# First batch of a fused attention, expert and mixing kernel: the gates of part 0 go through all their steps alone, parts 1 and 2 follow between the first masks, and a weight product moves behind the first increments

## The reference

```python
f = 1.0 / (1.0 + np.exp(-f_logit))                     # layer 1: gated linear attention
state = f[:, :, t, :, None] * state + einsum('bhd,bhe->bhde', k[:, :, t], v[:, :, t])
y[:, :, t] = einsum('bhd,bhde->bhe', q[:, :, t], state)
...
# layer 2: 4 experts of causal softmax attention (q, k, v of width 64), top 2 of 4 per token
# layer 3: theta = x @ w_theta; y = w_tok_r @ (x cos theta) + w_tok_i @ (x sin theta)
#          u = x + y; out = u + relu(u @ w_ch)
```

## Time and profile before

| | |
|---|---|
| median of 3 runs | 611.98 us (611.74 to 612.78) |
| profiled execution, its own time | 614.31 us |
| its span | 612.6 us, mean granted TensorE clock 0.989 |
| PE busy | 569.5 us, 93% of the span |
| DVE, ACT, POOL busy | 61%, 49%, 21% |
| chain that ended last | PE 77%, ACT 10%, DVE 8% |

### The profile page before, as it was taken

How to read it: one execution, slowest core, us unless ns; L and a number is a source line. 1 busy time by engine, 2 the same in 40 slices (tenths; PEclk the granted TensorE clock), 3 DMA queues, 4 the chain that set the end, 5 groups by cost and what they waited for, 6 DMA issues and landing times.

```text
span 612.6 us, 13201 instructions
## 1 busy us (share of the span) xinstructions
PE 569.5 (93%) x5532; PEld 526.5 (86%) x5532; DVE 376.0 (61%) x695; ACT 301.3 (49%) x623; POOL 127.5 (21%) x87
## 2 busy tenths in 40 slices
PE   0979899989899998999998989999999999999997
PEld 0779778889678987888996879999999999999997
DVE  2977868667776686766476757755344543455324
ACT  5658586645667366653357736523341233224211
POOL 1003440402340004400022314701320131012210
PEclk9999999999999998999998989999999999999999
DMA  8937020043110070000520000001000100010002
GB/s 284 308 114 285 26 53 27 2 137 150 53 53 2 7 281 0 2 1 4 217 95 1 2 1 1 1 2 69 10 1 1 51 27 1 1 52 27 0 1 78
DMA packets 17966, 37.19 MB, mean 61 GB/s; under 512 B 2160, under 2 KB 10608, under 8 KB 17392
## 3 DMA queue, kind: packets, MB, share of 16 engines
q1 hardware_dynamic: 17904, 36.32, 17.2%
HBM read 31.46 MB, written 4.72 MB: 59 GB/s over the span
## 4 chain that ended last, share of the span: by engine, by line
PE 77%; ACT 10%; DVE 8%; issue 2%; DMA 1%; SPq 0%; DVEq 0%; ACTq 0%
PE bank L1142 17%; PE bank L1143 17%; PE bank L1144 17%; PE bank L1341 5%; ACT prob L696 5%; PE bank L1368 4%; PE bank L1315 4%; PE bank L1160 3%; PE bank L1240 2%; DVE nmax L1043 2%; PE bank L1236 2%; PE bank L1207 1%; PE bank L1419 1%; PE bank L1221 1%; DMA gate<-fT 1%
## 5 line engine op out<-in xcount | busy, mean ns | idle before, releaser
L1142 PE MATMUL bank<-z_h,wt_h 128*128 128x384 f32 x288 | 98.1, 340 | 1.8 <-DVE z_l L871 1.8
L1143 PE MATMUL bank<-z_l,wt_h 128*128 128x384 f32 x288 | 97.8, 339 | 0.0
L1144 PE MATMUL bank<-z_h,wt_l 128*128 128x384 f32 x288 | 96.9, 337 | 0.0
L696 ACT ACTIVATE prob<-bank,nmax 128x384 f32<-128x384 f32 (+5 forms) x96 | 60.0, 631 | 28.4 <-DVE nmax L1043 28.3
L1043 DVE TENSOR_REDUCE nmax<-bank 128x1 f32<-128x384 f32 (+5 forms) x96 | 55.1, 619 | 27.1 <-PE bank L1321 19.6
L494 POOL TENSOR_TENSOR trig<-trig,x 128x768 f32<-128x768 f32 x18 | 33.5, 1862 | 152.1 <-ACT trig L588 92.7
L886 DVE TENSOR_SCALAR turns<-bank 128x384 int32<-128x384 f32 x22 | 12.2, 557 | 73.1 <-PE bank L1144 73.1
L1142 PEld LDWEIGHTS bank<-z_h,wt_h 128*128 128x128 f32 x288 | 54.1, 188 | 2.5 <-issue 2.2
L1143 PEld LDWEIGHTS bank<-z_l,wt_h 128*128 128x128 f32 x288 | 54.4, 189 | 0.0
L1144 PEld LDWEIGHTS bank<-z_h,wt_l 128*128 128x128 f32 x288 | 54.3, 189 | 0.0
L1341 PE MATMUL bank<-ident,prob 128*128 128x128 f32 x336 | 48.3, 290 | 4.5 <-ACT portion L711 3.9
(11 more groups left out here) (177 smaller groups left out, 1402.2 us busy)
## 6 DMA issues: line engine op xcount, KB each, us to landing
V<-v SPq DMA_DIRECT2D x4, 1152.0 KB, 10.1
gate<-fT SPq DMA_DIRECT2D x12, 384.0 KB, 3.2
q<-qT SPq DMA_DIRECT2D x12, 384.0 KB, 5.9
k<-kT SPq DMA_DIRECT2D x12, 384.0 KB, 6.4
wt_raw<-w_tok SPq DMA_DIRECT2D x6, 768.0 KB, 8.2
out<-x SPq DMA_DIRECT2D x24, 192.0 KB, 1.9
gate<-fT SPq DMA_DIRECT2D x3, 512.0 KB, 6.2
q<-qT SPq DMA_DIRECT2D x3, 512.0 KB, 9.6
```

What stands on the lines that cost most here:

```text
L696: nc.scalar.activation(prob[:, m % 2, r, at], bank[r][:, at], ACT.Exp, bias=nmax[:, m, k:k + 1], accum_out=den[:, m // 2, which, e:e + 1]) ...
L1142: nc.tensor.matmul(o, a_h, b_h, start=start, stop=False)
L1143: nc.tensor.matmul(o, a_h, b_l, start=False, stop=False)
L1144: return nc.tensor.matmul(o, a_l, b_h, start=False, stop=stop)
```

## The change

It reorders instructions on ACT, DVE and PE, and adds no arithmetic. ACT: part 0 goes through Exp and Ln alone; then Exp of part 1, Exp of minus the sum and Exp of the sum of part 0, Exp of part 2, Ln of parts 1 and 2; part 0's chunk decays come behind the first `kTs` copy, the rest of part 1 behind them. DVE: the scan of part 0 ahead of part 2's clamp; the scan of part 1 between the masks of chunks 0 and 1; q and k of part 1 and the scan of part 2 behind the first state; k of part 2 a chunk earlier. PE: `theta_weights` behind `turn_k(1)`, bank 5 first, bank 4 after ACT has copied the first outputs out of it. The second batch's clamps and Exps: two of four move from chunk 3 to chunk 4, the others behind the copies and splits of the transposed `xn`.

```diff
+            exp_first(0)
+            log_first(0)
+            exp_first(1)
             shrink_first(0)
             grow_first(0)
-            shrink_first(1)
-            act.wait_ge(wth_mm, 1)
-            nc.scalar.copy(staged(W_OTH, 768, 2), bank[2]...).then_inc(wth_copied, 1)
-            grow_first(1)
+            exp_first(2)
+            log_first(1)
+            log_first(2)
...
+                        if it < 1 and c == 0:      # ACT, behind the copy kTs of chunk c
+                            decay_chunks(chunks_of(0))
+                            shrink_first(1)
+                        if it < 1 and c == 2:
+                            shrink_first(2)
+                            grow_first(2)
...
                             if c == 1:             # ACT, behind the copy xn of chunk c - 1
-                                shrink_first(2)
-                                grow_first(2)
+                                grow_first(1)
+                                act.wait_ge(wth_mm, 1)
+                                nc.scalar.copy(staged(W_OTH, 768, 2), bank[2]...).then_inc(wth_copied, 1)
...
-                            elif c in (4, 5):
-                                exp_gates(it + 1, range(2 * c - 8, 2 * c - 6))
+                            elif c == NT - 1:
+                                exp_gates(1, (0, 1))
...
                         if it < 1:                 # ACT, behind the copies of the transposed xn
-                            log_gates(it + 1)
+                            exp_gates(1, (2, 3))
+                            log_gates(1)
...
+            clamp_first(0)                         # DVE
+            clamp_first(1)
             dve.wait_ge(consts, 13)
             scan_first(0)
-            scan_first(1)
+            clamp_first(2)
             scale_first_q(0)
             scale_first_k(0)
-            scale_first_q(1)
...
                 mask(0)
                 if it < 1:
-                    scale_first_k(1)
+                    scan_first(1)
...
                         if c == 0:                 # DVE, behind the state of chunk c
+                            scale_first_q(1)
+                            scale_first_k(1)
                             scan_first(2)
                         elif c == 1:
                             scale_first_q(2)
                             worst_sum(0)
-                        elif c == 2:
                             scale_first_k(2)
-                        elif c in (3, 4):
-                            clamp_gates(1, 2 * c - 6)
-                            clamp_gates(1, 2 * c - 5)
+                        elif c == NT - 2:
+                            clamp_gates(1, 0)
+                            clamp_gates(1, 1)
...
+                if it < 1:                         # DVE, behind the splits xT_l, ahead of the copies Vm
+                    clamp_gates(1, 2)
+                    clamp_gates(1, 3)
...
-            pe.wait_ge(w_in[3], 32)                # PE, ahead of scores(0, 0)
-            for a in range(2):
-                for c in range(NC):
-                    mm = theta_weights(a, c)
-            mm.then_inc(wth_mm, 1)
...
-                if it < 1:
-                    pe.wait_ge(wth_copied, 1)
                 outputs(0)
                 increments(0)
                 turn_k(1)
+                if it < 1:
+                    pe.wait_ge(w_in[3], 32)
+                    for a in (1, 0):
+                        if a == 0:
+                            pe.wait_ge(x_copied, 1)
+                        for c in range(NC):
+                            mm = theta_weights(a, c)
+                    mm.then_inc(wth_mm, 1)
```

More of the change, by code:

```diff
@@ L602, in grow_first, with exp_first, log_first @@
                 nc.scalar.activation(gate[:, :, part(n)], gate[:, :, part(n)], ACT.Exp).then_inc(grown, 1)
-                decay_chunks(chunks_of(n))
-            for n in range(PARTS):
+                if n >= 1:
+                    decay_chunks(chunks_of(n))
+            def exp_first(n):
                 act.wait_ge(clamped, n + 1)
                 nc.scalar.activation(gate[:, :, part(n)], gate[:, :, part(n)], ACT.Exp, scale=-1.0).then_inc(expf, 1)
-            for n in range(PARTS):
+            def log_first(n):
                 act.wait_ge(expf, n + 1)
                 nc.scalar.activation(gate[:, :, part(n)], gate[:, :, part(n)], ACT.Ln, bias=1.0).then_inc(logf, 1)
+            exp_first(0)
+            log_first(0)
+            exp_first(1)
             shrink_first(0)
             grow_first(0)
-            shrink_first(1)
-            act.wait_ge(wth_mm, 1)
-            nc.scalar.copy(staged(W_OTH, 768, 2), bank[2][:, :].rearrange("p (a n) -> p a n", a=2)[:, :, 0:D]
-                           ).then_inc(wth_copied, 1)
-            grow_first(1)
+            exp_first(2)
+            log_first(1)
+            log_first(2)
             for it in range(B):
@@ L632, in recurrence_copies @@
                             if c == 1:
-                                shrink_first(2)
-                                grow_first(2)
+                                grow_first(1)
+                                act.wait_ge(wth_mm, 1)
+                                nc.scalar.copy(staged(W_OTH, 768, 2), bank[2][:, :].rearrange(
+                                    "p (a n) -> p a n", a=2)[:, :, 0:D]).then_inc(wth_copied, 1)
                             elif c == 3:
@@ L898, in z_lo, with clamp_first @@
                 lo(z_l[:, s, :, :], trig_of(b, s), z_h[:, s, :, :], zl_done)
-            for n in range(PARTS):
+            def clamp_first(n):
                 dve.wait_ge(f_in[n], 16)
@@ L1258, in _ @@
                         increments(c)
+                    if it < 1 and c == 1:
+                        pe.wait_ge(wth_copied, 1)
                     outputs(c)
```

## The result

The changed kernel takes 615.58 us (median of 17 runs, 612.89 to 617.33), the kernel before 611.74 in the runs beside it (17 runs, 610.89 to 614.08): a ratio of 1.0059, 95% interval 1.0048 to 1.0071, or 3.6 us slower (the medians differ by 3.8). The forecast was 612.4 with a range to 614.4, so it is missed on the slow side.

What follows compares the result with a forecast made beforehand. PE's chain was taken to bound most of the span. Last outputs −0.2 and second-batch gates +0.5 gave +0.3 to +0.4 us on 614.31, so 614.7, or 612.4 for the median; range 610.8 to 614.4.

Steps and rivals of the forecast that it cites:

- What the moved second-batch gates cost: Second batch: late clamps and Exps delay Ln 2.9 us, 1.81 covered; last QK split and first row maximum 0.5 us later.
- The clamps take 1.21 us as before: DVE, second batch: the two moved clamps keep their old duration, 1.21 us, behind the last xn split.
- POOL's answer: Ahead of DVE's comparison: POOL's reduction ends 6.25 us after worst, upper bound 8.1; comparison at 40.65.
- rival A: PE's early wait for V drops the clock to half pace between 20 and 28 us: +1.1 to +1.9 us; chance 0.25.
- Scores 0 at 15.5: PE, head: scores 0 start at about 15.5 instead of 21.85, 6.4 us earlier, behind DVE's k.
- V bounds turn_k(0): PE, head: V lands at 21.2, so turn_k(0) goes at 21.35 instead of 23.84; only 2.5 us are left.
- The product at 3.84 us in two pieces: PE, weight product between turn_k(1) and scores 2: starts 24.05, takes 3.84 us, its second half waiting for ACT's first xn copy.
- The chain through the table load: ACT and DVE from turn_k(0) through the third Exp load to part 1's k: scores 2 at 28.8, 2.2 us later.
- Both waits gone at scores 4: PE: idles of 0.91 and 0.94 us between scores 2 and 4 go; scores 4 start at 36.65 instead of 36.28.
- rival B: POOL's reduction result comes at the upper bound, comparison at 42.5: +1.6 and +0.5 us, 614.1; chance 0.07.
- C: Faster rival: PE keeps its 2.5 us and all three waits go, 610.1 or 610.6; sign a comparison before 39.9; chance 0.12.
- The gain at the last outputs, −0.2: PE, end of the early stage: last outputs at 44.7, 0.2 us earlier than before.

Runs made afterwards that it cites:

- e2: The changed kernel, with POOL starting its subtraction for wqk_l only after all four second-batch clamps; 611.58 us, ratio 0.9995 to the kernel before.
- e3: The kernel before with only the moves of the second batch's clamps and Exps; 613.62 us, ratio 1.0037 to the kernel before.
- e1: The changed kernel with all four second-batch clamps at chunk NT − 2, two Exps still late; 611.33 us, ratio 0.9988 to the kernel before.
- e5: The changed kernel with POOL's subtraction for wqk_l cut into three instructions of 128x512; 613.9 us, ratio 1.0032 to the kernel before.
- e8: The changed kernel run again with no edit; 614.42 us, ratio 1.004 to the kernel before, nine runs.
- e10: e1 with worst (the maximum over the chunk sums) ahead of q of part 2 on DVE; 611.19 us, ratio 0.9996 to the kernel before.
- e11: e1 with V's transfer ahead of part 1's q and k, and worst ahead of q of part 2; 610.28 us, ratio 0.9977 to the kernel before.
- e12: The kernel before with only V's transfer moved ahead of q and k of part 1; 610.92 us, ratio 0.9988 to the kernel before.
- e4: The changed kernel with the second batch's clamps and Exps back where the kernel before has them; 612.67 us, ratio 1.0017 to the kernel before.
- e6: e1 with part 0's decays and the third Exp load ahead of the first kTs copy; 610.77 us, ratio 0.9991 to the kernel before.
- e7: e6 with V's transfer ahead of part 1's q and k, and worst ahead of q of part 2; 608.82 us, ratio 0.9947 to the kernel before, six runs.
- e9: e1 with V's transfer issued ahead of part 1 of q and k; 610.71 us, ratio 0.9976 to the kernel before.

## Why the prediction was wrong

**The step that failed** stands in "What the moved second-batch gates cost": "The clamps take 1.21 us as before". The prediction carried a duration over from a place where POOL was idle to one where POOL runs its subtraction for wqk_l. The direction of the term was right and its size was not: 0.5 us forecast, 2.86 in the profile. e2 takes away only the overlap and leaves 0.6, so the term was right without it. e3 shows the loss without the rest of the change, e1 the rest without the loss. No rival named it: all five looked at PE, ACT, V or POOL's answer ahead of 47 us.

**The mechanism.** In three kernels a clamp ended 0.41 to 0.43 us behind the end of the POOL instruction in whose time it began: after 53.49 behind 53.07 (50.26 + 3.229; 49.60 + 3.47), e3 51.90 behind 51.48 (48.37 + 3.530; 48.01 + 3.47), e5 50.00 behind 49.58 (49.31 + 0.689; 48.30 + 1.279). In e8, after's second profile, it is 52.82 behind 52.40. A slowdown in proportion would not end at a fixed distance from POOL's end. So all of the clamp but some 0.2 us (its 0.61 less the 0.42 behind POOL's end) has to wait while the POOL instruction runs. The Trainium skill, SBUF — State Buffer, Who interferes with whom, says that a tensor_scalar in its two-port mode takes a pair of ports that DVE shares with POOL, and that whoever issues first has it for the whole instruction; the trace agrees with that rule in the numbers just given, though no row names the mode in which the clamp ran. It also says that a DVE instruction with at most one input in SBUF outside that mode does not contend, and the trace agrees there too: in after DVE's xT_l splits (one input in PSUM) go on at 0.55 us each while POOL runs.

**The second part of the loss.** Between the two profiles 2.4 of the 3.6 us are the later softmax job. The rest is put down to the clock. Windows of after from 71 us (length, busy and count of PE, PEld, DVE, ACT, POOL, then the granted clock, DMA share, GB/s):

```profile
71.00:74.40 3.40, 0.33 (x8) 0.19 (x7) 3.40 (x7) 1.47 (x5) 2.80 (x2) 1.00 0.00 0
74.40:78.00 3.60, 3.27 (x24) 2.22 (x25) 1.96 (x5) 2.39 (x9) 3.60 (x3) 0.71 0.39 109
```

and of e2 in the second of these stretches:

```profile
74.40:78.00 3.60, 2.97 (x35) 2.12 (x33) 2.27 (x5) 3.60 (x10) 0.75 (x1) 1.00 0.41 109
```

After a wait of 3.07 us the mean grant falls to 0.71, which is a mixture of the 2.4 and the 1.2 GHz level; e8 (0.57) and e3 (0.50) show the same. Behind the shorter wait, about 1.3 us, it may fall (0.52 in before's profile, and in e1, e10, e11 and e12) or not (1.00 in e2's, and in e4, e6, e7 and e9). So the long wait seems to make certain what otherwise happens in some executions. The runs fit: no execution of after or of e3 (wait 3.07 us) has a mean of 0.997, while some of before, e1 and e2 (about 1.3 us) and of e5 (2.02) do. After's mean over 26 runs is 0.9915 against 0.9945, one step of 0.003, and so some 1.0 us (an estimate). With 2.4 that makes 3.4 of the 3.6. It is rival A's mechanism at another place: the prediction priced it for the head alone. That the wait causes the fall is argued from this coincidence; no run varied the wait alone.

Two things bound this account. Each profiled execution's own time less the start of its softmax job takes only few values: 540.0 to 540.1 us in after, e2, e5, e7, e10, e11 and e12, 540.8 in e4, e6 and e9, 541.6 in e8, 542.3 in e1, 542.4 in before and 543.1 in e3. The granted clock goes with them: before's profile has four stretches at the lower level (from 73, 240, 326 and 360 us), after's two (from 75 and 243), e8's three and e4's two. By these differences a stretch costs some 0.8 to 1.1 us (an estimate: e8 less e4 0.8 for one, before less after 2.3 for two; after with two and e2 with one are level, so which stretch it is counts too). No other effect of the change shows behind the job, and after's profile has the span of before's because it had two such stretches fewer. And before's profile started late, so the job is more than 2.4 us later against a usual execution: 3.4 us in after and 2.8 in e8 against e12's 70.89. So how the 3.6 us divide between the later job and the clock is open: 2.4 and 1.0, or some 3 and the rest.

**Point by point, the rest.**
- Scores 0 at 15.5: right (15.51). It ran at half pace, 3.79 us for 32 matmuls that took 2.06 before, since PE had done nothing ahead of it (3.77 to 3.79 in every profile with this head, 2.06 in every one with the product first); V's wait hid it.
- V bounds turn_k(0): right, but at 20.20, not 21.35. V was issued at 8.27 us instead of 9.19; in e3, with before's order on SP's queue, it was issued at 8.01. In e3 and e12, which keep before's head, the third clamp came at 8.66 and 8.81 and scores 0 at 20.57 and 20.71, in before's profile at 9.95 and 21.85: that execution had its gates late, and the forecast was built on it. e4 has turn_k(0) at 20.20 too.
- The product at 3.84 us in two pieces: right in size in both profiles (4.04; 2.10 and 2.20). In the first it came later, because PE was still at half pace (turn_k(0) took 1.12 us against 0.66); so rival A's half pace is there in some executions, though its sign, a granted clock of 0.5 before 28 us, is not (1.00 from 20 to 28). What it costs is the 1.0 us between the two profiles' scores 2, within the 0.7 to 1.5 that A gave for them.
- The chain through the table load: its length is right, its number in the first profile is luck. From turn_k(0) to scores 2 the forecast has 7.45 us; e8, where k of part 1 ends at 27.61, has 7.43. In after's first profile it is 8.56, since k was done at 28.18 and PE, slow, was at scores 2 only at 28.76. V 1.15 us too early and a PE 1.1 us too slow cancel, and the later points, down to the comparison, inherit the hit. The activation behind the load began 0.01 us after it, so the further 1.38 us that the Trainium skill states (ScalarE: Activation LUTs, What ACT_TABLE_LOAD costs) did not come.
- Both waits gone at scores 4: right (36.51, forecast 36.65).
- POOL's answer, a delay of 6.25 us and not 8.1: right (6.38 in after, from worst's end at 33.92 to the reduction's at 40.30, and 6.29 in e8). The comparison went at 40.34 behind POOL (forecast 40.65), with an idle of 0.27; rival B is out. C's sign, a comparison before 39.9, did not come in this profile but did in e8 of the same kernel (39.68, with worst ended at 33.36). C's time did not: its last outputs are at 43.77, level with e12's 43.87, and 614.42 us is slower than before.
- The gain at the last outputs, −0.2: −0.50 between the two profiles, but before's was late itself. Of kernels that differ in the head alone, e3 (old head) has 42.54 and after, e8 and e2 have 44.43, 43.77 and 43.42: the new head is 0.9 to 1.9 us later there. What the profile showed as a small gain is the sum of this loss, of the two clamps that no longer stand ahead of the comparison, and of before's late start. e4's 1.0017, with those clamps back, says the same.

## What to carry to other kernels

A duration from the trace holds only beside the same neighbours: ask what the other engines run where an instruction is moved to, and for an in-place tensor_scalar on DVE look at POOL's timeline first. A short instruction that can be held up by a long one belongs before it, or the long one behind a semaphore (e2), not in between. When two profiles have the same span, compare their granted clock before believing it, and check a first event (here the first clamps) of the one profile against several executions.

## What was not expected of the hardware

- A 0.61 us clamp (128x768, SBUF to SBUF) took 3.23 and 3.53 us, up to 5.8 times, beside one POOL subtraction of 3.47 us; a scan of the same shape lost 0.17 (1.92 against 1.75) in e2, where POOL ran into its first 0.31 us. That is no milder effect: the clamps too lost some 0.2 us less than POOL still had to run.
- At the start PE ran at half pace while the granted clock read 1.00 (15 to 24.7 us of after's first profile): the granted clock does not show an engine that is not yet up to its pace, the durations do.
- V's transfer ahead of part 1's q and k may make the kernel before faster as well (0.9988, interval to 0.9999), though turn_k(0) does not wait for V there. Its last outputs in e12, 43.87 against 44.93, do not show it: scores 0 are 1.14 us earlier there because the third clamp is, 8.81 against 9.95, and e3 with V in its old place has both as early.
